# Channel attention and two MLPs on one core: each matmul of the MLPs issued as two of half the columns

## The reference

```python
q, k, v: (1, 6016, 256)
qn = q / (norm(q, axis=1) + 1e-06)
kn = k / (norm(k, axis=1) + 1e-06)
s = kn.transpose(0, 2, 1) @ qn / tau
a = exp(s - s.max(-1))
a /= a.sum(-1) + 1e-09
x = v @ a
h = x @ w_in1;  x = (h * cos(h)) @ w_out1
h = x @ w_in2;  y = (h * 1 / (1 + exp(-h))) @ w_out2
```

## Time and profile before

| | |
|---|---|
| runs of the kernel | 1125.93 and 1124.79 us, median 1125.36 |
| profiled execution, span from first to last instruction | 1123.1 us |
| the same execution, time outside the span | some 2 us: the two runs less the span are 1.7 and 2.8 us |
| PE (matmuls) busy | 1108.1 us, 4952 matmuls |
| PEld (weight loads) busy | 917.3 us, 4952 loads |
| DVE busy | 551.9 us |
| ACT busy | 578.9 us |

### The profile page before, as it was taken

The page is one execution under the profiler, slowest core; times in us unless marked ns, Lnnn a source line. Parts: engine busy times, 40 slices in busy tenths (PEclk is TensorE's granted clock), DMA queues, the critical chain, the costliest instruction groups (busy, mean ns, idle before and its releaser), DMA issues.

```text
span 1123.1 us, 12484 instructions
## 1 busy us (share of the span) xinstructions
PE 1108.1 (99%) x4952; PEld 917.3 (82%) x4952; DVE 551.9 (49%) x505; ACT 578.9 (52%) x604; POOL 0.8 (0%) x7
## 2 busy tenths in 40 slices
PE   7999999999999999999999999999999999999998
PEld 7978788888888888888888888888888888889888
DVE  8879852562462463364265255256246346326312
ACT  7777753554554454355455455355455445446443
POOL 0000000000000000000000000000000000000000
PEclk9989999999999999999999999999999999999999
DMA  8823000000000000000000000000000000000000
GB/s 286 285 95 96 36 1 19 20 1 19 19 0 19 0 19 19 0 19 0 19 19 0 19 19 0 19 19 0 19 19 0 14 0 19 0 1 20 1 19 15
DMA packets 15539, 33.31 MB, mean 30 GB/s; under 512 B 1184, under 2 KB 5792, under 8 KB 15520
## 3 DMA queue, kind: packets, MB, share of 16 engines
q1 hardware_dynamic: 15520, 33.03, 8.7%
HBM read 26.87 MB, written 6.16 MB: 29 GB/s over the span
## 4 chain that ended last, share of the span: by engine, by line
PE 98%; DVE 1%; DMA 0%; ACT 0%; issue 0%; DVEq 0%
PE h_ps L638 16%; PE h_ps L639 16%; PE h_ps L637 16%; PE x_ps L637 8%; PE x_ps L638 8%; PE x_ps L639 8%; PE y_ps L638 8%; PE y_ps L637 8%; PE y_ps L639 8%; PE x_ps L652 2%; PE h_ps L654 1%; PE h_ps L656 1%; DMA qk_raw<-qk 0%; DVE qk_lo L457 0%; DVE work L510 0%; DVE work L517 0%
## 5 line engine op out<-in xcount | busy, mean ns | idle before, releaser
L498 DVE TENSOR_TENSOR g_lo<-work,g_hi 128x1024 fp32r<-128x1024 f32 (+1 forms) x192 | 230.4, 1200 | 285.1 <-ACT g_hi L378 273.0
L510 DVE SCALAR_TENSOR_TENSOR work<-work,h_ps 128x1024 f32<-128x1024 int32 (+1 forms) x96 | 115.1, 1199 | 156.4 <-ACT work L361 156.3
L361 ACT ACTIVATE work<-h_ps 128x1024 int32<-128x1024 f32 (+1 forms) x96 | 96.9, 1010 | 167.3 <-PE h_ps L639 167.2
L378 ACT ACTIVATE g_hi<-h_ps 128x1024 fp32r<-128x1024 f32 (+1 forms) x96 | 96.8, 1008 | 160.0 <-PE y_ps L639 124.7
L376 ACT ACTIVATE work<-h_ps 128x1024 f32<-128x1024 f32 (+1 forms) x96 | 96.8, 1008 | 135.8 <-PE h_ps L639 135.8
L637 PE MATMUL x_ps<-g_hi,w1out_hi 128*128 128x512 f32 (+1 forms) x384 | 150.0, 391 | 0.4 <-DVE x_lo L484 0.4
L638 PE MATMUL h_ps<-v_lo,wu_hi 128*128 128x512 f32 (+1 forms) x384 | 149.8, 390 | 0.0
L639 PE MATMUL h_ps<-v_hi,wu_lo 128*128 128x512 f32 (+1 forms) x384 | 149.8, 390 | 0.0
L638 PE MATMUL x_ps<-g_lo,w1out_hi 128*128 128x512 f32 (+1 forms) x384 | 149.8, 390 | 0.0
L637 PE MATMUL h_ps<-v_hi,wu_hi 128*128 128x512 f32 (+1 forms) x384 | 149.5, 389 | 0.0
L639 PE MATMUL x_ps<-g_hi,w1out_lo 128*128 128x512 f32 (+1 forms) x384 | 149.2, 389 | 0.0
(11 more groups left out here) (111 smaller groups left out, 1151.4 us busy)
## 6 DMA issues: line engine op xcount, KB each, us to landing
qk_raw<-qk SPq DMA_DIRECT2D x23, 512.0 KB, 4.7
v_raw<-vT SPq DMA_DIRECT2D x11, 512.0 KB, 3.8
yT<-y_out SPq DMA_DIRECT2D x11, 512.0 KB, 2.8
w_raw<-w_in SPq DMA_DIRECT2D x8, 512.0 KB, 5.4
w_raw<-w_out SPq DMA_DIRECT2D x8, 512.0 KB, 4.0
v_raw<-vT SPq DMA_DIRECT2D x1, 384.0 KB, 3.3
yT<-y_out SPq DMA_DIRECT2D x2, 192.0 KB, 1.9
qk_raw<-qk SPq DMA_DIRECT2D x1, 256.0 KB, 4.6
```

The costliest lines, as they stand in the source:

```text
L361: nc.scalar.activation(work_int[:, slot, :, 0:n], h, ACT.Identity, bias=0.25).then_inc(turns_ready, 1)
L378: nc.scalar.activation(g_hi[:, slot, :, 0:n], h, ACT.Silu).then_inc(g_hi_ready, 1)
L498: nc.vector.tensor_tensor(g_lo[:, slot, :, 0:n], work[:, slot, :, 0:n], g_hi[:, slot, :, 0:n], ALU.subtract).then_inc(g_ready, 1)
L510: nc.vector.scalar_tensor_tensor(out=work[:, slot, :, 0:n], in0=work_int[:, slot, :, 0:n], scalar=0.25, in1=h, op0=ALU.subtract, op1=ALU.s ...
```

## The change

`three_passes` issues each of its matmuls twice, on the first and on the second half of the columns: first all three passes of the first half, then all three of the second. Only the very first matmul of an accumulator's group has the start flag, and only the very last the stop flag. The functions that call it are as they were, and the last matmul is still the one that counts up the semaphore. So 512 columns become twice 256, and in the last tile 384 become twice 192, each half with a load of the same weights.

```diff
                 def three_passes(out, w_hi, w_lo, m_hi, m_lo, start, stop):
-                    nc.tensor.matmul(out, w_hi, m_hi, start=start, stop=False)
-                    nc.tensor.matmul(out, w_hi, m_lo, start=False, stop=False)
-                    return nc.tensor.matmul(out, w_lo, m_hi, start=False, stop=stop)
+                    half = out.shape[1] // 2
+                    for a in (0, half):
+                        cols = slice(a, a + half)
+                        nc.tensor.matmul(out[:, cols], w_hi, m_hi[:, cols], start=start and a == 0, stop=False,
+                                         skip_group_check=True)
+                        nc.tensor.matmul(out[:, cols], w_hi, m_lo[:, cols], start=False, stop=False,
+                                         skip_group_check=True)
+                        mm = nc.tensor.matmul(out[:, cols], w_lo, m_hi[:, cols], start=False, stop=stop and a > 0,
+                                              skip_group_check=True)
+                    return mm
```

## The result

| | before | changed |
|---|---|---|
| median | 1125.36 us | 1147.78 us (1147.48 and 1148.09) |
| ratio to before | | 1.020, 95% interval 1.017 to 1.023 |
| profiled span | 1123.1 us | 1145.7 us |
| matmuls, and as many loads | 4952 | 9608 |

The account below looks back on a forecast made before the run. PE was taken as saturated, time being matmuls times their distance. 1123.1 us span + 56.4 (37.6 for 512-wide matmuls, 18.8 for the last tile) + 2.3 around the span gave 1182 us, +5.0%; range 1140 to 1240.

Parts of the forecast that it names:

- What bounds the kernel: Whole kernel: PE alone is saturated, so time is the number of matmuls times the distance between their starts.
- The last tile: 384 matmuls halved to 192 columns: 112 ns a pair, bound by loads (otherwise 93.3 or 120), +18.8 us.
- The argument from the eight one-column matmuls: Eight loads, each with a one-column matmul, span 0.97 us: a load step takes 111 ns, which 192 columns can't cover.
- The first term of the sum: Fold and eleven full tiles: 4272 matmuls of 512 columns become two 120 ns pairs instead of 231.2 ns, +37.6 us.
- The price of a pair: Each load and matmul pair loses a fixed 13.3 ns or so, sometimes 20, beyond its columns: 120 ns for 256.
- Its lower bound: A 256-wide pair takes at least about 117 ns, read from the score chunk's own 256-wide matmul.
- Rival A: Loss grows with columns, not per load: 1142 us, or 1156 with the narrow tile bound by loads; chance 0.15.
- its two signs: What would decide for loss growing with columns: 256-wide pairs in the loop at 117 ns or less, narrow ones below 100.
- Rival B: Loads and matmuls hinder each other in both halves: 126.7 ns a pair, 1245 us (half of it 1212); chance 0.22.
- Rival C: Doubled loop program no longer stays loaded; each of eight back edges waits for a transfer: +24 us, 1206 us; chance 0.08.
- the sequencer: PE's instruction issue: at most 38 ns per instruction where a 120 ns pair needs one each 60 ns; put at nothing.
- The half clock of the fold: Stretch at 1.2 GHz: two halves take what the whole takes; under 1 us if loads were late.

Follow-up runs that it names:

- padded pair of kernels: 192 unused bytes a partition behind the small tiles, added to the kernel before (nothing split): 1104.36 us; and to the changed kernel (all split): 1178.81 us.

## Why the prediction was wrong, point by point

- **What bounds the kernel**: right. PE stayed busy, its idle time stayed at 15 us, the chunks kept their 467 ns a round, and the time was the number of pairs times their distance.
- **The last tile**: right. The step "the last tile becomes bound by loads: 112 ns a pair" measured 110.6, and its +18.8 us measured +19.0 when done alone. Its other values, 93.3 and 120, are ruled out. The argument from the eight one-column matmuls held down to 96 columns (111 ns) as long as the clock was full.
- **The first term of the sum**: this is the step that failed. "I take 120" measured 116.0 on average, so the term 4272 x 8.8 = +37.6 us was in truth 4272 x 0.8 = 3, and 4.0 when measured alone. The price of a pair was read as fixed, "about 13.3 ns, sometimes 20", and the 20.0 of the hidden half was treated as a nuisance beside the rule. It was the clue. Whole matmuls on tiles that don't lie alike lose up to 20.0 ns, but their halves lose between 6.6 and 11.2 in the changed kernel (113.3 to 117.9 less 106.7), so that two halves cost on average a little less than the whole did (230.0 against 233.3, 231.2 against 231.7). Only the second MLP's output, which lies alike, lost about what was forecast for a divided matmul: 10 ns against 8.8. That the two effects all but cancel in this layout was in no step of the forecast; why halves lose less than wholes on tiles that don't lie alike stays open. The fixed 13.3 holds exactly where weights and columns lie alike: 226.7 for 512 columns, 120.0 for 256. In the padded pair of kernels the forecast's rule gives, after the fact, 4272 x 13.3 = +57 us and +19 for the last tile, 76 us, and 74 were measured.
- **Its lower bound**, 117 by the chunk's 256-wide matmul, was no bound: 113.3 occurs.
- **Rival A** was nearest in time (1142, or 1156 with the narrow tile bound by loads). Of its two signs one came, 116.0 in the loop, and the other, narrow pairs below 100, didn't. Its idea, a loss that grows with the columns, fits the average of the loop (two halves 232.0 against 231.2) but is not what happens: the padded kernels lose the same 13.3 at 512 and at 256 columns.
- **Rival B** didn't come, though the range reached to it. It expected loads and matmuls to be in each other's way more with loads under every column; the worst pair seen at the full clock in a settled stretch was 120.0.
- **Rival C and the sequencer**: rightly small. 26 blocks were fetched where 14 were, each once, and no hole stands at the back edge; PE's idle time is that of before.
- **The half clock of the fold** cost nothing, as said. Of a clock that falls while narrow matmuls run the forecast had no word; at 192 columns it didn't happen; at 96 the kernel was 232 us slower, 129 more than the 103 that loads at the full clock would have cost.

The measured 1148 us lies in the range of 1140 to 1240, but not by the forecast's merit: the range reached down that far for rival A. The change was 22.4 us where 56.4 was forecast, and the whole gap lies in the first term.

## What to carry to other kernels

When TensorE is saturated, measure the distance between the starts of matmuls kind by kind, and compare it with columns / 2.4 GHz; different distances for the same width are a sign that can be worth more than any change in the order of the work (here 1.9% for 192 unused bytes, all weight and column tiles beginning alike within 512 bytes). A price per instruction that was read from one width and one layout must not be carried to another without asking why it differs between kinds. And at the full clock a matmul with its own 128 x 128 float32r weight load hardly gets cheaper below 256 columns (113 to 120 ns there, 110.6 at 192, 111 at 96); a tail tile should be kept as wide as it can be.

## What was not expected of the hardware

- The distance of matmuls depends on how the weights and the streamed columns lie to each other in SBUF. Alike within 512 bytes, it is 226.7 ns for 512 columns and 120.0 for 256 with no variation between kinds; at the other offsets tried (128, 192, 320 and 384 bytes) the mean of a block is between 230 and 234, or between 113.3 and 118.5. That both read the same memory at the same moment and hinder each other would explain it, but that was argued, not shown. Alike tiles were tried at three places (448, 128 and 0 bytes behind a multiple of 512), each time with 226.7 ns once settled, so it is the relation and not the address. A step of 128 bytes is excluded by the kernel with 64 unused bytes; whether it is 512 or 256 stays open.
- At the half clock matmuls of 256 columns or more lose nothing: their distances are columns / 1.2 GHz. In the kernels with 192 unused bytes the fold has the same 427 ns for 512 columns and 213 for 256, so the layout doesn't matter there.
- Whether a layout exists in which halves all take 113.3 ns, and why blocks of one kind take 113.4 and 117.9 in turn, wasn't found out.
- With matmuls of 96 columns the granted clock fell to 0.50 for most of the last tile, with PE busy throughout, and their distance went from 111 to 213 ns; in the same place with 192 columns the clock stayed at 1.00.
